# A complex recurrent mixer and two gated MLPs on one core: transposes, scores and outputs of each chunk in slots of their own, one product pair a slot earlier

## The reference

```python
def _attn_ref(q, k, v, a_re, a_im):
    mag = np.sqrt(a_re * a_re + a_im * a_im)
    scale = np.minimum(mag, 0.999) / (mag + 1e-06)
    a_re_n, a_im_n = (a_re * scale, a_im * scale)
    for t in range(S):
        ar, ai = (a_re_n[:, :, t, :, None], a_im_n[:, :, t, :, None])
        new_re = ar * S_re - ai * S_im
        new_im = ar * S_im + ai * S_re
        kv = np.einsum('bhd,bhe->bhde', k[:, :, t], v[:, :, t])
        S_re, S_im = (new_re + kv, new_im)
        y[:, :, t] = np.einsum('bhd,bhde->bhe', q[:, :, t], S_re)

def _moe_ref(x, w_in, w_out):              # w_in 384x2048, w_out 2048x384
    h = x @ w_in
    return (h * np.clip(h + 3.0, 0.0, 6.0) / 6.0) @ w_out

def _moe2_ref(x, w1, w2, w3, w_out):       # w1, w2 384x1024, w3 1024x1024, w_out 1024x384
    return ((x @ w1) * (x @ w2) @ w3) @ w_out
```

## Time and profile before

| | |
|---|---|
| median of 3 runs | 985.01 us (984.34 to 985.52) |
| the profiled execution's own time | 984.38 us |
| its span, first to last instruction | 982.5 us |
| TensorE busy | 892.5 us (91%) |
| DVE, ACT, POOL busy | 490.4 us (50%), 431.4 us (44%), 263.2 us (27%) |
| mean granted TensorE clock | 0.973 |
| unit 0 begins at | 100.1 us |
| units 1 to 6 begin at | 192.0, 267.2, 338.2, 410.2, 481.4, 554.5 us |
| unit 7; the second MLP begins | 620.9 us; 674.1 us |

### The profile page before, as it was taken

One profiled execution on the slowest core, in us unless ns is written; L12 is line 12 of the kernel. 1 busy time (PEld: TensorE's weight loads), 2 busy tenths in 40 slices (PEclk: granted clock), 3 DMA queues, 4 the chain that ended last, 5 costly groups with the idle time before them and its releaser, 6 DMA issues.

```text
span 982.5 us, 14750 instructions
## 1 busy us (share of the span) xinstructions
PE 892.5 (91%) x5721; PEld 815.1 (83%) x5721; DVE 490.4 (50%) x669; ACT 431.4 (44%) x653; POOL 263.2 (27%) x200
## 2 busy tenths in 40 slices
PE   6954678889999898999888999999999999999996
PEld 3544678888999788999888999998888888888886
DVE  6538759769668678678678532252111111111110
ACT  5544564664574565565565422453222222222121
POOL 1012345222222322222322322352222121213121
PEclk9987788999999999999999999999999999999998
DMA  9594232353443443532632520701001010101001
GB/s 351 199 261 127 78 58 79 115 100 94 114 93 102 114 85 94 129 87 78 138 82 73 99 74 17 266 1 57 1 14 51 5 60 1 65 1 65 1 33 35
DMA packets 64473, 85.86 MB, mean 87 GB/s; under 512 B 6928, under 2 KB 50576, under 8 KB 64400
## 3 DMA queue, kind: packets, MB, share of 16 engines
q1 hardware_dynamic: 64400, 84.87, 31.5%
HBM read 45.22 MB, written 11.01 MB: 57 GB/s over the span
## 4 chain that ended last, share of the span: by engine, by line
PE 46%; issue 25%; POOL 10%; DVE 7%; ACT 4%; SPq 4%; DMA 3%; POOLq 0%; DVEq 0%; ACTq 0%
PE hb L950 10%; POOL gL L1352 9%; PE acc L972 8%; PE acc L829 5%; PE hb L809 5%; PE bQ L950 5%; PE bR L950 5%; PE bP L972 3%; DMA F<-QKs 2%; PE acc L903 2%; PE hb L903 1%; SPq L349 1%; DVE g_sb L1261 1%; DVE QKc L1209 1%; PE bQ L859 1%
## 5 line engine op out<-in xcount | busy, mean ns | idle before, releaser
L1352 POOL TENSOR_TENSOR gL<-g_sb,gH 128x384 fp32r<-128x384 f32 x128 | 160.3, 1253 | 387.5 <-ACT gH L1048 383.6
L809 PE MATMUL hb<-xHL,winH 128*128 128x384 f32 x768 | 164.8, 350 | 19.5 <-DMA xHL<-yHL 11.6
L809 PEld LDWEIGHTS hb<-xHL,winH 128*128 128x128 f32 x768 | 134.1, 192 | 24.7 <-DMA xHL<-yHL 13.3
L1261 DVE SCALAR_TENSOR_TENSOR g_sb<-t_sb,hb 128x384 f32<-128x384 f32 x128 | 70.3, 549 | 154.6 <-ACT t_sb L1058 135.0
L1048 ACT CAST gH<-g_sb 128x384 fp32r<-128x384 f32 x128 | 65.8, 514 | 173.0 <-DVE g_sb L1261 173.0
L829 PE MATMUL acc<-gH,woutH 128*128 128x384 f32 x384 | 130.4, 339 | 2.5 <-POOL gL L1352 1.4
L829 PE MATMUL acc<-gH,woutL 128*128 128x384 f32 x384 | 129.4, 337 | 0.0
L829 PE MATMUL acc<-gL,woutH 128*128 128x384 f32 x384 | 129.3, 337 | 0.0
L1365 POOL TENSOR_TENSOR pL<-p_sb,pH 128x512 fp32r<-128x512 f32 x48 | 67.0, 1396 | 231.9 <-ACT pH L1109 231.9
L1058 ACT ACTIVATE t_sb<-hb,cst 128x384 f32<-128x384 f32 x128 | 74.0, 578 | 77.8 <-PE hb L809 77.6
L809 PE MATMUL hb<-xHL,winL 128*128 128x384 f32 x384 | 89.2, 340 | 0.0
(11 more groups left out here) (160 smaller groups left out, 1732.3 us busy)
## 6 DMA issues: line engine op xcount, KB each, us to landing
xHL<-yHL SPq DMA_DIRECT2D x48, 144.0 KB, 2.7
QKs<-in_qk_x_dram SPq DMA_DIRECT2D x8, 768.0 KB, 4.6
F<-QKc SPq DMA_DIRECT2D x16, 292.5 KB, 5.2
F<-QKs SPq DMA_DIRECT2D x16, 292.5 KB, 6.2
AR<-in_a_re_x_dram SPq DMA_DIRECT2D x8, 576.0 KB, 3.7
AI<-in_a_im_x_dram SPq DMA_DIRECT2D x8, 576.0 KB, 4.8
v_sb<-in_v_dram SPq DMA_DIRECT2D x24, 192.0 KB, 2.6
x_dram<-x_sb SPq DMA_DIRECT2D x24, 192.0 KB, 3.8
```

Of the source, the lines that this page charges most:

```text
L809: mm = pe.matmul(o, w[:, kk * DF1 + ft * P:kk * DF1 + (ft + 1) * P], xv(u)[:, 2 * kk + part, :], start=(i == 0), stop=(i == 8))
L1261: dve.scalar_tensor_tensor(out=g_sb[:, :], in0=t_sb[:, :], scalar=6.0, in1=hb[n % 2][:, 0:UNIT], op0=ALU.min, op1=ALU.mult).then_inc(s["hs ...
L1352: pool.tensor_tensor(gL[:, (n % 3) * UNIT:(n % 3 + 1) * UNIT], g_sb[:, :], gH[:, (n % 3) * UNIT:(n % 3 + 1) * UNIT].bitcast(F32), ALU.subt ...
```

## The change

In units 1 to 6 the transposes of the third chunk move from slot 9 to slot 10, and the scores of all three chunks from slots 2, 6, 10 to slots 3, 7, 11. The outputs stay in slots 4, 8, 12. And on DVE the cosine products of two chunks move from step 12 to the end of step 11, in all units. Nothing is added or taken away.

```diff
             if not -1 <= u < NU - 1:
                 return None
-            at_ = STAGE.get(u, ((1, 5, 9), (2, 6, 10), (4, 8, 12)))[("TK", "S", "YU").index(stage)]
+            at_ = STAGE.get(u, ((1, 5, 10), (3, 7, 11), (4, 8, 12)))[("TK", "S", "YU").index(stage)]
             return CPU * (u + 1) + at_.index(sl) if sl in at_ else None
...
                     dve.wait_ge(s["last_dma"], 16 * (p + 1))
                     for i, grow in enumerate((AI, AR)):
                         dve.tensor_tensor(last(part(QKs, i)), last(part(QKs, i)), last(tokens(grow)), ALU.mult).then_inc(s["last_decayed"], 1)
-                if t == 12:
                     dve.wait_ge(s["pair_decayed"], 2 * (p + 1))
                     dve.wait_ge(s["cos_turns"], p + 1)
                     for i in range(2):
                         dve.tensor_tensor(pair(part(QKc, i)), pair(part(QKs, i)), pair(tokens(W2)), ALU.mult).then_inc(s["pair_cos"], 1)
+                if t == 12:
                     dve.wait_ge(s["sin_turns"], p + 1)
                     for i in range(2):
                         dve.tensor_tensor(pair(part(QKs, i)), pair(part(QKs, i)), pair(tokens(W3)), ALU.mult).then_inc(s["pair_sin"], 1)
```

## The result

The changed kernel takes 992.4 us in the median of 7 runs (989.16 to 994.79), the kernel before 984.34 us beside it (980.63 to 985.52): a ratio of 1.0092, 95% interval 1.007 to 1.0113. It is 8 us slower. The forecast of 987.6 us had the sign and not the size; the range of 980 to 993 us holds the result at its edge. The profiled execution took 992.4 us, with a span of 990.6 us (982.5 before) and a mean granted clock of 0.957 (0.973 before).

A forecast was written before the change was run, and what follows sets the result against it. The prediction took chains of DVE and ACT, not TensorE's waits, to bound the units. Its terms came to -3.4 us without the clock and +6 for it: +2.6 us on a median of 985.01, so 987.6 us, range 980 to 993.

The forecast's parts named there:

- No wait for F, and the new waits: TensorE, units 1 to 6: F's 8.9 us wait goes; new waits of 2 to 3.8 us in slots 8, 11, 12.
- The ends of the chains: DVE and ACT set the ends: slot 12 in units 1, 3, 5 2.0 us later, units 2 and 4 1.4 us.
- D: Start of DVE's gate product of slot 4; predicted sooner by 4.2 us in units 1, 3, 5 and 0.6 in 2, 4.
- the steps: Terms for units 1 to 6 without clock: +1.9 (units 1, 3, 5), +2.2 (2, 4), -1.2 (6), -1.4 (gate product before unit 1).
- The early gain in unit 0: Unit 0: cosine pair runs in DVE's idle time, scores at 125.9 and not 130.83 us, -4.9 us.
- The clock: TensorE, units 1 to 5: clock falls in four or five long waits, 1.2 to 1.7 us each, +6 us, bounds 0 and 8.5.
- rival 2: The clock falls after slot 8's waits too, in five units: +4 us on the forecast, 991.7 us, chance 0.1.
- the -3.4 us without the clock: Whole kernel, sum of all terms but the clock: 1.9 + 2.2 - 1.2 - 4.9 - 1.4 us.
- Rival 1: TensorE's clock stays up at the long waits: -3.4 us, 981.6 us, faster, chance 0.2.
- Rival 3: Unit 0's early gain is absent, its scatter held by something else such as SP's queue: 992.5 us, chance 0.08.
- Rival 4: DVE's and ACT's chains have unseen slack, so the 8.9 us wait for F is simply saved: 976 us, chance 0.07.
- 4.2, 0.6 and 1.2 us: Predicted gains: D sooner in units 1, 3, 5 (4.2) and 2, 4 (0.6); unit 6 keeps the wait for F (1.2).

The follow-up runs named there:

- the filled kernel: Useless products put ahead of slot 11 scores, slot 12 outputs and slot 8 outputs in units 1 to 5 of the changed kernel: 981.39 us.

## Why the prediction was off, step by step

**No wait for F, and the new waits: right.** Computed were three waits of 3.6 us at slot 11, five of 2 us at slot 8 and two of 3.8 us at slot 12. Measured were 3.57, 3.57 and 2.77; 1.92 to 2.06; 3.10 and 3.91 us. The two shorter ones of the long kind stand in units 2 and 5, where the clock had fallen at slot 8 and TensorE came later.

**The ends of the chains: right.** With the clock filled up (so that it is not in it), slot 12 of units 1, 3 and 5 starts at D + 38.44 (computed D + 38.57), and the unit behind 2 and 4 at D + 52.55 (computed D + 52.6; the terms as written add up to 52.45). In units 2 to 5 D itself came somewhat sooner than computed: against the unit's start it moved by -0.77 and -0.93 us in units 2 and 4 for the computed -0.18 and -0.47, and by -1.33 and -2.13 in units 3 and 5 for -1.03 and -1.85; in unit 1 it moved by -2.26 for -2.69. Units 1 to 6 together gave -0.5 us without the clock, where the steps had +1.5.

**The early gain in unit 0: wrong step.** "The copies [are ready] at 124.1, so nothing else is late next" is the sentence that failed. The sine pair ended at 117.06, as computed (117.2), and F would have let the scores go near 126; the run with the split moved shows F landing 25.4 us behind the unit's start, for a computed 25.8. But I took the third chunk's sine products as short. GpSimd's split of woutL, which waits for ACT, moved with them (from 122.17 to 119.52 us), and DVE stayed held: 5.12 us, the copies done at 127.1. DVE's timeline of the kernel before had it:

```profile
121.03 5.11 DVE L1218 TENSOR_TENSOR QKs<-QKs,W 128x384 f32<-128x384 f32 x2
```

I had read the hold of the cosine pair by the first split, and not asked what the second one would hold. Ten profiles with the pair moved and that split in place have unit 0 at 89.1 to 90.6 us, in the median 90.1: a gain of 1.9 us, not 4.9.
The Trainium skill, "SBUF — State Buffer", section "SBUF: two separate sides", says that a VectorE operation with two inputs in SBUF and a GpSimd operation that reads SBUF take one pair of ports exclusively, and whichever starts second is blocked till the first is done. The trace agrees: POOL's split ran from 119.52 to 123.08 us, and of DVE's two products, begun at 118.38, the second began at 119.67 and ended at 123.50.

**The clock: the term that was mis-sized.** It was +6 us with bounds of 0 and 8.5; it was 11 to 11.5 us, outside its bounds. Three things were in it. The five long waits did fall, all of them, in this execution (about 1.5 us each, 7.5 us: the upper part of what I had reckoned). Two of the stretches lasted twice as long, which added 1.2 us each; the one row that I priced from the earlier trace rows had shown a single one. And "of the waits in slot 8 I expect nothing on the path" was wrong: two of the five fell, at 0.9 us each, which is the size that rival 2 gave them. Rival 2, at 991.7 us, is near the result by its number only: its share of the 8 us is 1.7.
The Trainium skill, "TensorE: Matmul & The Clock Gate", section "HAM oscillation — how this bites in real kernels", has waits between groups of matmuls start each next group cold. By it the prediction's clock term was 8.5 and not 6 us, with all five falls, and this trace has all five. Other runs here show waits of 3.57 and 3.90 us without a fall, so it doesn't happen every time, and the two falls at slot 8 aren't foretold by it.

**The sum.** Added are 5.5 us of clock and 3.6 of unit 0 (1.34 us gained here, for 4.9); against them stand 2.0 us in units 1 to 6, and 0.95 us because unit 0 itself began sooner (it begins at 97.8 to 100.3 us in the fourteen profiles, so that is chance): 2.6 + 5.5 + 3.6 - 2.0 - 0.95 = 8.75 us at the start of unit 7, measured 8.68. The second MLP gave back 0.6. So the -3.4 us without the clock looks confirmed by the filled kernel (981.39 - 984.34 = -2.95 us), and it is partly luck: one step 3 us too good, others 2 us too bad. What is open is why unit 0 keeps only 1.9 of the 2.6 us by which its scores come sooner against its start, and why an equal wait lowers the clock in one unit and not in the next.

**The rivals.** Rival 1 (the clock stays up) had its price right: the filled kernel is that case, 981.4 for 981.6 us. Rival 3's 992.5 us is the nearest number to the result, and its observation came for the most part (1.3 of the 4.9 us were there), with another cause: DVE and not SP's queue. Its number is right by luck, since it has the clock at 6 us. Rival 4 falls for the change: with F's wait down to 0.5 us, the time went to the next chain. For the first chunk's move by itself it does not fall so far: that move gains 8.5 us (976.49 to 967.99), 6.5 of it in units 1 to 6 of the two profiles, where 6.2 us of waits for F and one low stretch go. The prediction's own terms for it, 4.2, 0.6 and 1.2 us, come to 6.0.

## What to carry to other kernels

Before a consumer is moved later to spare it a wait, look for what its product is queued behind on the engine that makes it, and what is queued behind the moved piece: here one slot put three small copies behind a table switch and two masks behind a 2.6 us pair, and 14 us of waits became 28 (all waits of TensorE together: 30 became 35, and the clock took another 11). Try such a table stage by stage. Two of its three moves were worth keeping or nearly free, and the third hid 24 us of loss behind their gain. And price a wait on TensorE's path twice, once as the wait, once as the slow stretch that may follow; if it can't be removed, useless products in it are cheap (110 of them, -11 us).

## What the runs showed of the hardware

- The clock falls with waits as short as 1.90 us, in 16 of 34 cases up to 2.14 us, with none of 148 up to 1.80 us, and with 22 of 26 from 2.77 us up. The wait's length alone doesn't decide: the same 3.9 us wait with and without a fall lie 146 us apart in one execution.
- One fall costs 0.85 us at slot 8, 1.5 to 1.6 us at slots 11 and 12, and 2.4 to 2.8 us where the stretch is double (five units in which a wait of 3.6 to 3.9 us has one). Why slot 8 is cheaper isn't shown; there may be slack behind it.
- A GpSimd operation on SBUF that splits a weight (3.5 us) lengthens the two short DVE products beside it from 1.82 to 5.12 us, step 0's first operation (1125) from 1.35 to 3.80 us, the cosine pair from 2.64 to 5.03 us and the sine pair from 1.81 to 5.07 us. Moving it by a slot moves the hold to the next operation. The shorter split gL does the same on a smaller scale: in the 2.64 and the 1.82 us one of the two products takes 1.77 for 0.94 and 1.35 for 0.55 us beside it.
